# Moving one PSUM bank from the score blocks to the transposed fills in a fused attention and mixture-of-experts kernel

## The reference

```python
scores = scale * np.matmul(q, k.transpose(0, 1, 3, 2))           # 4 batches, 8 heads, 576 x 576
decay = cum[:, :, :, None] - cum[:, :, None, :]                   # cum = cumsum(log(clip(f)))
scores = np.where(causal, -1e9, scores + decay)
attn = np.exp(scores - np.max(scores, axis=-1, keepdims=True))
attn = attn / (np.sum(attn, axis=-1, keepdims=True) + 1e-09)
x = np.matmul(attn, v)                                            # then (tokens, 512)
h = x @ w_in; g = where(h >= 1, h, where(h <= -1, 0, (h + 1) ** 2 / 4)); x = g @ w_out
# then each of 2304 tokens goes to one of 8 experts: relu(x @ w1[e]) @ w2[e], times a gate
```

## Time and profile before

| | us |
|---|---|
| median of three runs | 856.62 (856.4 to 856.82) |
| the profiled execution's own time | 856.74 |
| its span in the profile | 854.5 |
| PE busy | 835.6 (98%) |
| DVE, ACT, POOL busy | 411.4, 395.5, 351.1 |

### The profile page before, as it was taken

The page is one execution under the profiler, slowest core; times in us unless marked ns, Lnnn a source line. Parts: engine busy times, 40 slices in busy tenths (PEclk is TensorE's granted clock), DMA queues, the critical chain, the costliest instruction groups (busy, mean ns, idle before and its releaser), DMA issues.

```text
span 854.5 us, 13804 instructions
## 1 busy us (share of the span) xinstructions
PE 835.6 (98%) x5018; PEld 781.9 (91%) x5019; DVE 411.4 (48%) x1002; ACT 395.5 (46%) x916; POOL 351.1 (41%) x366
## 2 busy tenths in 40 slices
PE   8999999999999999999999999999999999999996
PEld 5888888889999999999999999999998998998985
DVE  6877888787554454444444445455525210210201
ACT  6777777777665534534534544443332121211221
POOL 5665678773766211111102201084311592010285
PEclk9999999999999999999999999999999999999999
DMA  6676888872100201211031023242323354213041
GB/s 223 192 222 221 261 276 264 277 218 75 56 1 1 102 30 55 84 47 56 17 101 41 29 102 105 74 149 62 85 76 111 110 161 135 82 42 124 26 138 40
DMA packets 70941, 95.62 MB, mean 112 GB/s; under 512 B 7174, under 2 KB 47110, under 8 KB 70864
## 3 DMA queue, kind: packets, MB, share of 16 engines
q1 hardware_dynamic: 62688, 80.33, 30.6%
q10 hardware_dynamic: 6416, 9.59, 3.2%
q0 software_dynamic: 1760, 4.72, 1.5%
HBM read 70.87 MB, written 24.27 MB: 111 GB/s over the span
## 4 chain that ended last, share of the span: by engine, by line
PE 91%; ACT 4%; DVE 1%; issue 1%; DMA 1%; SPq 0%; POOL 0%; POOLq 0%; ACTq 0%
PE psum L1508 24%; PE psum L1510 24%; PE psum L1509 24%; PE psum L1479 5%; PE psum L1462 5%; PE psum L1435 4%; ACT pr L848 2%; ACT pth L858 2%; PE psum L1440 1%; DVE ptl L1118 1%; DMA qraw<-q 1%; PE psum L1591 1%; PE psum L1575 0%; PE psum L1576 0%; PE psum L1415 0%
## 5 line engine op out<-in xcount | busy, mean ns | idle before, releaser
L1508 PE MATMUL psum<-xh,winh 128*128 128x384 f32 x384 | 129.1, 336 | 0.0
L1508 PE MATMUL psum<-gh,wouth 128*128 128x384 f32 x384 | 128.3, 334 | 0.2 <-issue 0.2
L1509 PE MATMUL psum<-xl,winh 128*128 128x384 f32 x384 | 128.4, 334 | 0.0
L1510 PE MATMUL psum<-xh,winl 128*128 128x384 f32 x384 | 128.4, 334 | 0.0
L1510 PE MATMUL psum<-gh,woutl 128*128 128x384 f32 x384 | 128.3, 334 | 0.0
L1509 PE MATMUL psum<-gl,wouth 128*128 128x384 f32 x384 | 128.3, 334 | 0.0
L882 ACT ACTIVATE hpos<-psum,minus 128x384 f32<-128x384 f32 x96 | 55.9, 582 | 142.3 <-DVE hclip L1144 142.1
L1149 DVE TENSOR_TENSOR g<-hpos,hsq 128x384 f32<-128x384 f32 x96 | 64.7, 674 | 109.0 <-ACT hsq L884 109.0
L675 POOL TENSOR_TENSOR xst<-xst 128x384 f32<-128x384 f32 x24 | 24.6, 1025 | 175.6 <-DMA xst<-rinv_d 175.6
L1254 DVE SCALAR_TENSOR_TENSOR hl<-psum,hh 128x384 fp32r<-128x384 f32 x48 | 26.8, 557 | 139.5 <-ACT hh L938 139.5
L1153 DVE TENSOR_TENSOR gl<-g,gh 128x384 fp32r<-128x384 f32 x96 | 64.1, 668 | 61.0 <-ACT gh L915 61.0
(11 more groups left out here) (233 smaller groups left out, 1863.5 us busy)
## 6 DMA issues: line engine op xcount, KB each, us to landing
praw<-moe_w SPq DMA_DIRECT2D x48, 256.0 KB, 2.7
qraw<-q SPq DMA_DIRECT2D x15, 448.0 KB, 4.6
vraw<-vk SPq DMA_DIRECT2D x16, 320.0 KB, 3.4
xh<-yh_d SPq DMA_DIRECT2D x20, 256.0 KB, 4.2
xl<-yl_d SPq DMA_DIRECT2D x20, 256.0 KB, 4.5
kraw<-k SPq DMA_DIRECT2D x16, 288.0 KB, 3.7
xa_d<-xo SPq DMA_DIRECT2D x16, 288.0 KB, 3.9
xb_d<-xo SPq DMA_DIRECT2D x16, 288.0 KB, 4.2
```

What stands on the lines that cost most here:

```text
L1508: nc.tensor.matmul(psum_at, ah, bh, start=start, stop=False)
L1509: nc.tensor.matmul(psum_at, ah, bl, start=False, stop=False)
L1510: return nc.tensor.matmul(psum_at, al, bh, start=False, stop=stop)
```

## The change

One bank goes from the scores to the fills: scores rotate over banks 0 to 2, fills over 3 to 5. Block 8 still takes two banks next to each other. Every wait follows: `score` waits for the minima of the block three slots before, `turn` for the subtraction of the fill three before. The turned inverses now lie in the third fill bank of the rotation, so their copy is awaited before fill 2 of the next pair and not before fill 1. Block 1's mask is held back behind block 2's products, as block 4's is behind block 5's. On DVE the minima of block 1' move from ahead of the subtractions of fills 2 and 3 to behind them. On ACT the casts of fills 4 and 5 move ahead of the exponential of block 1'. The dense layer's units 0 and 1 wait for one block more.

```diff
-    CASTS_FIRST = 5
+    CASTS_FIRST = (5, 7)
...
-        PT, PX, PY = (4, 5), 6, 7
+        SCORES, PT, PX, PY = 3, (3, 4, 5), 6, 7
...
+        def score_banks(p, i):
+            if i == NB - 1:
+                return (p % 2, p % 2 + 1)
+            return (((0, 2, 1), (2, 0, 1))[p % 2][i % SCORES],)
+        def minimum_ahead(p, i):
+            last = (NB + 1) * p + i + (i == NB - 1) - SCORES
+            return NB * (last // (NB + 1)) + min(last % (NB + 1), NB - 1) + 1 if last >= 0 else 0
...
+        def fill_bank(p, k):
+            return PT[(FILLS * p + k) % len(PT)]
...
-                if i != CASTS_FIRST and 0 <= n + 2 < STEPS:
+                if i not in CASTS_FIRST and 0 <= n + 2 < STEPS:
                     exp(n + 2)
                 if 0 <= n - 1 < STEPS:
                     for k in fills_of(i):
                         high(p, k)
-                if i == CASTS_FIRST and 0 <= n + 2 < STEPS:
+                if i in CASTS_FIRST and 0 <= n + 2 < STEPS:
                     exp(n + 2)
...
-                nc.vector.tensor_copy(rturn[:, p % 2, :], psum[0:NB, PT[1], P:2 * P]).then_inc(r_copied, 1)
+                nc.vector.tensor_copy(rturn[:, p % 2, :], psum[0:NB, fill_bank(p + 1, FILLS - 1), P:2 * P]).then_inc(r_copied, 1)
...
-                m = tile_of(n + 3)[1]
-                if m != 1 and 0 <= n + 3 < STEPS:
+                if 0 <= n + 3 < STEPS:
                     masked(n + 3)
-                if m == 0 and 0 <= n + 4 < STEPS:
-                    masked(n + 4)
...
-            MASK_LATER = (4,)
+            MASK_LATER = (1, 4)
...
-                last = 10 * p + i + (i == NB - 1) - 4
-                if last >= 0:
-                    pe.wait_ge(lowest, NB * (last // 10) + min(last % 10, NB - 1) + 1)
-                bank = (10 * p + i) % 4
+                if minimum_ahead(p, i):
+                    pe.wait_ge(lowest, minimum_ahead(p, i))
+                banks = score_banks(p, i)
...
-                if FILLS * p + k >= 2:
-                    pe.wait_ge(pt_l, FILLS * p + k - 1)
-                if k == 1 and p >= 2:
+                if FILLS * p + k >= len(PT):
+                    pe.wait_ge(pt_l, FILLS * p + k - len(PT) + 1)
+                if k == len(PT) - 1 and p >= 2:
                     pe.wait_ge(r_copied, p - 1)
...
                     if u < EARLY:
-                        pe.wait_ge(lowest, STEPS - 2 + u)
+                        pe.wait_ge(lowest, STEPS - 1 + u)
```

More of the change, by code:

```diff
@@ L375, in stacked, with of_bank @@
             return bass.AP(full.tensor, full.offset, [[full.ap[0][0], P], [ROW, nb], [1, ni * P]])
-        def of_bank(k):
+        def fill_bank(p, k):
+            return PT[(FILLS * p + k) % len(PT)]
+        def of_bank(p, k):
             _, b, nb, i, ni = FILL[k]
-            full = psum[:, PT[k % 2], 0:nb * ni * P]
+            full = psum[:, fill_bank(p, k), 0:nb * ni * P]
             return full if nb == 1 or i < 4 else full.rearrange("p (b c) -> p b c", b=nb)
@@ L857, in high @@
                 rows = D if k == FILLS - 1 else P
-                nc.scalar.copy(stacked(pth, k)[0:rows], of_bank(k)[0:rows]).then_inc(pt_h, 1)
+                nc.scalar.copy(stacked(pth, k)[0:rows], of_bank(p, k)[0:rows]).then_inc(pt_h, 1)
             def copy_early(p):
@@ L1087, in masked @@
                     dve.wait_ge(exped, NB * (p - 1))
-                bank = (10 * p + i) % 4
+                banks = score_banks(p, i)
                 out_at, c_at = pr[:, at_tile(i):at_tile(i) + w], c8[:, p % 2, 0:w]
                 if i < NB - 1:
-                    src = psum[:, bank, 0:w]
+                    src = psum[:, banks[0], 0:w]
                 else:
-                    src = psum[:, bank:bank + 2, 0:w // 2]
+                    src = psum[:, banks[0]:banks[1] + 1, 0:w // 2]
                     out_at = out_at.rearrange("p (a c) -> p a c", a=2)
@@ L1114, in low @@
                     last = stacked(pth, k)
-                    nc.vector.tensor_tensor(last[D:P], of_bank(k)[0:D], last[0:D].bitcast(F32),
+                    nc.vector.tensor_tensor(last[D:P], of_bank(p, k)[0:D], last[0:D].bitcast(F32),
                                             ALU.subtract).then_inc(pt_l, 1)
                 else:
-                    nc.vector.tensor_tensor(stacked(ptl, k), of_bank(k), stacked(pth, k).bitcast(F32),
+                    nc.vector.tensor_tensor(stacked(ptl, k), of_bank(p, k), stacked(pth, k).bitcast(F32),
                                             ALU.subtract).then_inc(pt_l, 1)
@@ L1405, in _ @@
                                  ident_b[:].unsqueeze(1).to_broadcast([P, 4, P]), start=True, stop=True)
-            MASK_LATER = (4,)
+            MASK_LATER = (1, 4)
             def mask(n):
                 p, i = tile_of(n)
-                bank, w = (10 * p + i) % 4, keys(i)
+                bank, w = score_banks(p, i)[-1], keys(i)
                 if i == NB - 1:
-                    bank, w = bank + 1, w // 2
+                    w = w // 2
                 nc.tensor.matmul(psum[:, bank, w - D:w], ident_b[:], mask_b[:], start=False,
@@ L1425, in score @@
                     pe.wait_ge(q_l, p + 1)
-                last = 10 * p + i + (i == NB - 1) - 4
-                if last >= 0:
-                    pe.wait_ge(lowest, NB * (last // 10) + min(last % 10, NB - 1) + 1)
-                bank = (10 * p + i) % 4
+                if minimum_ahead(p, i):
+                    pe.wait_ge(lowest, minimum_ahead(p, i))
+                banks = score_banks(p, i)
                 passes = ((qh, kh), (qh, kl), (ql, kh))
                 if i < RAW:
-                    nc.tensor.matmul(psum[:, bank, 0:w], qf[:, p % 2, i, :], kf[:, p % 2, 0:w], start=True, stop=False)
+                    nc.tensor.matmul(psum[:, banks[0], 0:w], qf[:, p % 2, i, :], kf[:, p % 2, 0:w], start=True, stop=False)
                 elif i < NB - 1:
                     for a, (q_, k_) in enumerate(passes):
-                        nc.tensor.matmul(psum[:, bank, 0:w], q_[:, p % 2, i - RAW, :], k_[:, p % 2, 0:w],
+                        nc.tensor.matmul(psum[:, banks[0], 0:w], q_[:, p % 2, i - RAW, :], k_[:, p % 2, 0:w],
                                          start=a == 0, stop=False)
@@ L1439, in score @@
                         for a, (q_, k_) in enumerate(passes):
-                            nc.tensor.matmul(psum[:, bank + j, 0:w // 2], q_[:, p % 2, i - RAW, :],
+                            nc.tensor.matmul(psum[:, banks[j], 0:w // 2], q_[:, p % 2, i - RAW, :],
                                              k_[:, p % 2, j * (w // 2):(j + 1) * (w // 2)],
@@ L1461, in turn @@
                         at = (b - b0) * ni + i - i0
-                        x = nc.tensor.transpose(psum[:, PT[k % 2], at * P:(at + 1) * P],
+                        x = nc.tensor.transpose(psum[:, fill_bank(p, k), at * P:(at + 1) * P],
                                                 pr[:, at_tile(i) + b * P:at_tile(i) + (b + 1) * P], ident[:])
@@ L1469, in turn_inverse @@
                 pe.wait_ge(inv_ok, p + 1)
-                return nc.tensor.transpose(psum[:, PT[1], P:2 * P], rinv[:, p % 2, :], ident[:])
+                return nc.tensor.transpose(psum[:, fill_bank(p + 1, FILLS - 1), P:2 * P], rinv[:, p % 2, :], ident[:])
             def head(p, h, i0, ni, dst, signal):
```

## The result

| | before | changed |
|---|---|---|
| median, us | 856.72 (856.4 to 857.6, 4 runs) | 849.44 (848.79 to 850.91, 4 runs) |
| ratio to before, 95% interval | | 0.9916 (0.9899 to 0.9933) |
| profiled execution, span | 854.5 | 847.3 |
| interval between scores 0', pairs without additions (third pair on) | 12.20 to 12.25 | 11.56 to 11.57 |
| the same, pairs with additions for the dense layer | 12.20 to 12.23 | 11.85 to 12.01, mean 11.89 |

A forecast was written before the change was run, and what follows sets the result against it. PE's waits for fill banks were taken to bound the kernel. Six intervals gaining 0.70 us and nine gaining 0.60 give 9.6, less 0.4 at the start: 9.2 us off, 847.4 us, range 844.0 to 851.5.

The forecast's parts named there:

- four waits for a bank of two: PE's waits ahead of fills 4, 6, 7 and 0' for the subtraction two fills before: 1.05 us a pair.
- Parts 1 to 4: One pair's new timetable on PE, ACT, DVE and the score banks: interval 11.50 us without additions, 11.60 with, from 12.20.
- both new waits: On PE: 0.27 us ahead of the late products, 0.08 or 0.18 us ahead of score 8'.
- part 2: ACT: the swap starts fill 4's cast at 2.73, pays only with the third bank; fill 6's cast 5.02, before 5.22.
- Part 4: Fourth score bank gone: score 8' waits for minima of 6', starting at 9.31 us, or 9.41 with additions.
- part 7: Start and last pair: score 3 falls behind the first wait, 0.4 us more (0 to 0.8); last pair 0.
- PE bound: Rival: casts overlap more, the new waits vanish, interval 11.15 us, time 841.3 us; chance 0.08.
- The score ring taking half: Rival: six handovers from minima to score 8' cost 0.05 us more each, 0.3 us an interval, 851.9 us; chance 0.15.
- Slower: Rival: the same ring's steps run end to end, score 8' at 10.4, interval 12.6, 863.0 us; chance 0.03.
- no effect: Rival: fills 4, 6 and 0' wait for something other than the bank, 856.6 us; chance 0.03.
- The rule of repeated gaps: Trainium skill: a repeating gap on the engine that should be saturated can mean too few buffers; here 1.05 us a pair.

The follow-up runs named there:

- three_scores_only: Kernel before with three score banks, bank 3 left unused, fills still in two banks, every order as before: 856.87 us against 856.47, ratio 1.0004.
- banks_alone: Changed kernel with all three moves of order undone (casts of fills 4 and 5, minima and mask of block 1'), only its banks kept: 848.89 us, ratio 0.9911.
- copies_later: Changed kernel with ACT's copy of early products behind casts of fills 6 and 7, DVE's copy of turned inverses behind minima of 4': 841.74 us, ratio 0.9822.
- swap_only: Kernel before, two fill banks, with only the casts of fills 4 and 5 moved ahead of the exponential of block 1': 858.28 us, ratio 1.0021.
- no_swap: Changed kernel with the casts of fills 4 and 5 again behind the exponential of block 1': 849.39 us, ratio to the kernel before 0.9926.

## Why the prediction was right, and where it was not

**What bounds it.** Right: four waits for a bank of two, fifteen times. Together they are 1.13 us and not 1.05, since fill 7's was 0.15. That the fourth score bank was free in the old timetable and the third fill bank is what was lacking is shown by three_scores_only (nothing) and banks_alone (everything).

**Parts 1 to 4.** The timetable holds to 0.1 us wherever it can be read, and so do both new waits: late products at t = 6.69 (6.79 said), score 8' at 9.35 (9.31). Without additions the interval is 11.56 where I said 11.50.

**The swap, part 2.** I wrote that the swap pays only with the bank and that the two need each other. The first half is right (alone it costs 1.8 us). The second is wrong: the bank doesn't need the swap. My own working had the reason in it, the exponential that is moved stands ahead of fill 6's cast in either order, but I credited the swap with the start of fill 4's cast without asking whether anything after it depended on that. It is worth 0.04 us a pair beside the other two moves and nothing without them (banks_alone); no timing here can tell either from nothing.

**Part 4, pairs with additions: the term that was mis-sized.** "In pairs with the additions not before 6.89 + 124.82 - 123.30" took DVE's subtraction at the 0.65 us that it had in the row, as though its length belonged to it. Free it costs DVE 0.47 us (118.88 to 119.35 in the short pair above); the rest was a collision with POOL's cast of q, whose end lay about 0.3 us after the subtraction's start. The change moves DVE from t = 7.50 to 7.28 while POOL's cast stays at 6.9 to 7.1, so the overlap grew to 0.56 us, and up to 0.71, and the cost to 0.88 and more: intervals of 11.89 on average in place of 11.60. Eight pairs by 0.29 are 2.3 us, somewhat more than the whole miss of 2.0. I also counted nine pairs with additions (7 to 15, in the description of the kernel too); there are eight (7 to 14), so of the fifteen intervals seven are without.

**Ends, part 7.** I took +0.4. In the two traces the third pair's score 0' comes 0.73 us earlier. The first traces differ for other reasons (scores start at 9.88 instead of 9.13, and the granted clock is 1.00 from 10 to 30 us instead of 0.91), so this says nothing of the third score bank's own price; three_scores_only, at +0.40 us with an interval from -0.4 to +1.1, allows both 0 and 0.4.

The sum, by the traces: 0.73 + 5 x 0.65 before the additions, 97.70 - 95.15 = 2.55 over the eight pairs with them, and 0.64 after: 7.2 us of span. The forecast's terms for these were 0.30 (0.70 less 0.4), 5 x 0.70, 8 x 0.60 and 0.70. The first came out 0.4 us better than forecast, by a difference that these two traces can't put down to the change; as far as it isn't the change's, it is luck, and without it the miss would be up to 2.5 us.

**The rivals.** PE bound needed the new waits to vanish; copies_later shows that bound, at 11.00. The score ring taking half came out at 0.06 us a pair of its 0.3. Slower and no effect are out. The rule of repeated gaps would have given all of the gap: it gave 0.65 of the 1.13 us, as another chain, 0.65 us shorter than the old interval, stood behind the banks.

## What to carry to other kernels

When a buffer is added, don't ask only which waits it removes; walk the next chain (here cast, subtraction, minima) in the new timetable and find where it catches the engine again, as it is there that the next edit belongs: two copies moved in order brought as much again (7.7 us) as the bank (7.3), and nothing at all without it. Take a bundle apart, since three of the four parts here were together worth nothing and one of them costs time by itself; but what a part is worth depends on what binds, as the held-back mask shows, whose 0.07 us count only once the chain is gone. And a duration read from a row is work only if nothing was shared: where DVE reads SBUF beside a busy POOL, look at which POOL instruction it overlaps before carrying its length to another moment.

## What the runs showed of the hardware

A blocked DVE or POOL instruction appears as a longer one and not as idle time. The same 128x384 subtraction from SBUF was shown with 0.54 or 0.55 us where it went first or met no POOL instruction, with 0.59 (swap_only) to 1.12 beside POOL's cast of q, with up to 1.68 beside its subtraction of k and up to 2.13 beside that of q; held up, it always lasted until POOL's instruction ended plus 0.40 to 0.42 us. In the other direction POOL's cast of q took 1.28 to 1.52 us in place of 0.94.

Who goes first decides a whole pair's length, 11.56 or 11.86, so that nearly equal kernels show both kinds. The shown starts tell it only roughly. POOL's cast won wherever it was shown at least 0.23 us ahead (118.67 against 118.90 in the changed kernel); at leads of 0.04 (three_scores_only), 0.08 and 0.10 (no_swap) and 0.18 us (banks_alone) DVE's subtraction kept its 0.54 us. POOL's subtractions won at shorter leads, that for k at 0.17 us and that for v, against `rden`, at 0.13 us (both copies_later).

Width doesn't protect an instruction: `rden`, nine columns and one SBUF operand, was shown with 0.17 us where it started near the end of POOL's subtraction for v and with 1.46 where it started 0.13 us behind that one's start. DVE's subtractions with one operand in PSUM and one in SBUF kept their 0.69 us.
